# Attention, MLP and gated MLP on one core: the memory term by halves of the rows, one scores tile fewer, and another order at both ends of the second MLP

## What is computed

```python
def _attn_ref(q, k, v, M_prev, z_prev, beta):        # B, H, S, D = 4, 8, 576, 64
    scores = (1 / sqrt(D)) * q @ k.T, masked above the diagonal
    a = exp(scores - scores.max(-1)); a /= a.sum(-1) + 1e-9
    local = a @ v
    q_p = np.where(q > 0, q, np.exp(q) - 1.0) + 1.0    # phi(q)
    mem_out = (q_p @ M_prev) / (q_p @ z_prev + 1e-6)
    g = 1 / (1 + exp(-beta))                           # one gate per head
    return g * mem_out + (1 - g) * local
def _moe_ref(x, w_in, w_out):                          # 2304 tokens, 512 -> 2048 -> 512
    h = x @ w_in
    return (h / (1 + exp(-h))) @ w_out
def _moe2_ref(x, w_in, w_out, g_ln):                   # 512 -> 1024 -> 512
    h = x @ w_in
    solu = h * softmax(h)
    ln = (solu - mean) / sqrt(var + 1e-6) * g_ln
    return ln @ w_out
```

## Time and profile before

| | |
|---|---|
| runs, us | 891.49, 893.80, 893.99 |
| the profiled execution, us | 890.32 |
| its span, first to last instruction, us | 888.5 |
| mean granted clock of TensorE | 0.975 |
| PE busy, 4736 matmuls | 844.1 us, 95% |
| DVE, ACT, POOL busy | 529.3, 407.2, 340.2 us |
| hardware DMA queue, share of 16 engines | 34.9% |
| chain that ended last | PE 64%, issue 26%, ACT 4%, DVE 3% |

### The profile page before, as it was taken

How to read it: one execution, slowest core, us unless ns; L and a number is a source line. 1 busy time by engine, 2 the same in 40 slices (tenths; PEclk the granted TensorE clock), 3 DMA queues, 4 the chain that set the end, 5 groups by cost and what they waited for, 6 DMA issues and landing times.

```text
span 888.5 us, 13414 instructions
## 1 busy us (share of the span) xinstructions
PE 844.1 (95%) x4736; PEld 719.4 (81%) x4736; DVE 529.3 (60%) x1034; ACT 407.2 (46%) x897; POOL 340.2 (38%) x350
## 2 busy tenths in 40 slices
PE   4877899999999999999999999999998999999997
PEld 2665788888788888788888889999996888888885
DVE  5888776776764656665565441244435666666663
ACT  4776667666656545555554434415201222222221
POOL 4777558657645455455364314223200000000000
PEclk8898699999999999999999999999999999999998
DMA  5222265676664445445534337333200000000000
GB/s 171 82 71 71 85 208 181 219 241 221 225 200 152 146 158 163 149 146 173 176 120 135 141 122 306 120 128 134 94 1 13 24 14 21 24 24 24 24 24 24
DMA packets 50888, 105.64 MB, mean 119 GB/s; under 512 B 10384, under 2 KB 21648, under 8 KB 50576
## 3 DMA queue, kind: packets, MB, share of 16 engines
q1 hardware_dynamic: 50384, 104.88, 34.9%
q10 hardware_dynamic: 448, 0.02, 0.0%
HBM read 83.39 MB, written 21.50 MB: 118 GB/s over the span
## 4 chain that ended last, share of the span: by engine, by line
PE 64%; issue 26%; ACT 4%; DVE 3%; POOL 1%; DMA 1%; SPq 0%; POOLq 0%; ACTq 0%
PE banks L1274 23%; PE banks L1286 21%; PE banks L1242 8%; PE banks L1223 5%; PE banks L1189 4%; ACT prob L693 2%; PE banks L1197 1%; PE banks L1192 1%; ACT pt_hi L699 1%; PE banks L1400 1%; DVE pt_lo L947 1%; POOL st L675 1%; DVE neg_max L930 1%; DMA z_row<-in_z_prev 1%; ACT x_half L705 0%
## 5 line engine op out<-in xcount | busy, mean ns | idle before, releaser
L1286 PE MATMUL banks<-g_hi,wr 128*128 128x512 f32 (+1 forms) x640 | 196.6, 375 | 2.0 <-POOL g_lo L619 1.1
L602 POOL TENSOR_SCALAR prob<-prob,inv_sum,gate_all 128x576 f32<-128x576 f32 (+2 forms) x144 | 109.7, 771 | 86.9 <-DVE inv_sum L941 86.9
L1286 PEld LDWEIGHTS banks<-g_hi,wr 128*128 128x128 f32 x640 | 118.5, 188 | 17.1 <-issue 2.9
L1274 PE MATMUL banks<-xc_hi,wr 128*128 128x512 f32 x384 | 128.9, 402 | 0.0
L947 DVE TENSOR_TENSOR pt_lo<-banks,pt_hi 128x512 fp32r<-128x512 f32 x144 | 85.1, 595 | 56.4 <-ACT pt_hi L699 55.8
L1286 PE MATMUL banks<-g_lo,wr 128*128 128x512 f32 (+1 forms) x320 | 117.7, 368 | 0.0
L619 POOL TENSOR_TENSOR g_lo<-gu,g_hi 128x512 fp32r<-128x512 f32 x48 | 62.1, 1293 | 90.6 <-ACT g_hi L739 90.4
L699 ACT ACTIVATE pt_hi<-banks 128x512 fp32r<-128x512 f32 x144 | 75.6, 526 | 41.2 <-PE banks L1223 39.6
L1242 PE MATMUL banks<-pt_hi,vm 128*128 128x320 f32 (+4 forms) x352 | 90.5, 289 | 4.1 <-DVE pt_lo L947 2.2
L675 POOL TENSOR_TENSOR st<-st 128x1 f32<-128x1 f32 x18 | 9.9, 551 | 217.3 <-DVE st L1120 217.3
L693 ACT ACTIVATE prob<-banks,neg_max 128x576 f32<-128x576 f32 (+2 forms) x144 | 78.2, 548 | 19.1 <-DVE neg_max L930 14.7
(11 more groups left out here) (119 smaller groups left out, 1784.2 us busy)
## 6 DMA issues: line engine op xcount, KB each, us to landing
wr<-split_w SPq DMA_DIRECT2D x96, 512.0 KB, 3.2
split_w<-wr SPq DMA_DIRECT2D x32, 512.0 KB, 4.0
k_raw<-in_k_t SPq DMA_DIRECT2D x16, 288.0 KB, 3.1
qn_raw<-in_q_n SPq DMA_DIRECT2D x16, 288.0 KB, 3.6
out<-o SPq DMA_DIRECT2D x18, 256.0 KB, 2.0
q_raw<-in_q_t SPq DMA_DIRECT2D x16, 256.0 KB, 2.7
vm_raw<-in_v_main SPq DMA_DIRECT2D x16, 256.0 KB, 2.5
wr_raw<-in_w_in SPq DMA_DIRECT2D x16, 256.0 KB, 3.1
```

The source lines that it names most:

```text
L602: pool.tensor_scalar(pr, pr, inv_sum[p % 2][:, columns(t, h)], gate, ALU.mult, ALU.mult).then_inc(prob_done, 1)
L1274: mm = pe.matmul(out_bank, w[:, a, k], x[:, k], start=(i == 0), stop=(i == 3 * KC - 1))
L1286: mm = pe.matmul(out_bank, w[:, a, k], g, start=(i == 0), stop=(i == 11))
```

## The change

Three things are changed, and small ones that follow from them.

1. **phi by the memory.** phi(q) is laid out with head 0 of a block's 64 tokens beside head 1, even blocks of tokens in rows 0 to 63 and odd ones in rows 64 to 127 (`qn_raw[P, 5, 2, D]`; five column blocks where 4.5 are filled, loaded by four DMAs in pieces of 256 bytes). Turned, the two heads lie on the two halves of the rows, as a third head of `pt_hi` and `pt_lo`; M is in one block of `vm` (11 blocks of 64 columns in place of 14). In `values` calls 0 and 2 first make the memory product of both heads, with 64 rows each, into both banks; the heads' own products add to it. Call 0 and call 2 so wait for both banks.
2. **Scores of tiles 1 and 0** are made in one go in step 5, tile 0 behind tile 1 in the same banks, with one mask product over 256 columns; `sums` takes both at once. Step 7 has no scores.
3. **Second MLP.** `EARLY` is 29 in place of 30. The wait for the first MLP's additions stands in `turn_ln(0)`, behind the first half of `hidden2(1)`. For the last tiles (n = 17) PE does hidden2(17) ahead of product(15), and turn_ln(16) between its halves.
4. In the alone stage PE turns a step's further units ahead of `values`; `TURN` has units 1 and 2 in step 6. `v_high` goes from step 7 to 8, both `v_low` to step 9, `q_high` from 3 to 1, `k_low` and `load_qk` from 6 to 5. The first two DMAs of the tail of q are issued by ACT's queue, beta by one DMA.

```diff
-SCORES = {0: 4, 1: 3, 3: 2, 5: 1, 7: 0}
-TILES = [4, 3, 2, 1, 0]
+SCORES = {0: 4, 1: 3, 3: 2, 5: 1}
+TILES = [4, 3, 2, 1]
-TURN = [[], [-3], [], [-2], [-1], [0], [1], [2, 3], [4, 5]]
+TURN = [[], [-3], [], [-2], [-1], [0], [1, 2], [3], [4, 5]]
-EARLY = 30
+EARLY = 29
...
             def load_qn(p):
                 if p:
-                    sp.wait_ge(norm_sum, p)
+                    sp.wait_ge(phi_sum, p)
+                    sp.wait_ge(phi_z, p)
+                else:
+                    sp.wait_ge(qn_zeroed, 1)
-                sp.dma_start(qn_raw[:], q_n[i]).then_inc(qn_in, 16)
                 for h in range(2):
-                    sp.dma_start(z_row[h * D:(h + 1) * D], z_prev[i:i + 1, h, :].broadcast_to([D, D])).then_inc(qn_in, 16)
+                    for par in range(2):
+                        sp.dma_start(qn_raw[par * D:(par + 1) * D, 0:5 - par, h], q_n[i, h * D:(h + 1) * D, par::2])\
+                            .then_inc(qn_in, 16)
+                sp.dma_start(z_row[:], z_prev[i:i + 1].rearrange("o h d -> o (h d)").broadcast_to([P, 2 * D])).then_inc(qn_in, 16)
...
             def scores(p, t):
-                    w = P * (t + 1)
-                    for n, (q, k) in enumerate(products):
-                        for h in range(2):
-                            r = slice(h * D, (h + 1) * D)
-                            pe.matmul(bank[b + h][:, 0:w], q[r, P * t:P * (t + 1)], k[r, 0:w], start=(n == 0), stop=False,
-                                      skip_group_check=True)
+                    for u, at in ((t, 0),) if t > 1 else ((1, 0), (0, 2 * P)):
+                        w = P * (u + 1)
+                        for n, (q, k) in enumerate(products):
+                            for h in range(2):
+                                r = slice(h * D, (h + 1) * D)
+                                pe.matmul(bank[b + h][:, at:at + w], q[r, P * u:P * (u + 1)], k[r, 0:w],
+                                          start=(n == 0 and u == t), stop=False, skip_group_check=True)
...
             def values(p, i):
                 h = i % 2
-                if i == 0:
-                    pe.wait_ge(v_split, 2 * p + 2)
                 if h == 0:
+                    pe.wait_ge(v_split, 2 * p + 2)
                     pe.wait_ge(pt_lo_done, NU * p + VALUES_NEED[i // 2])
-                if 4 * p + i >= 2:
-                    pe.wait_ge(x_done, 4 * p + i - 1)
+                    pe.wait_ge(x_done, 4 * p + i)
+                    for pt in (pt_hi, pt_lo):
+                        for g in range(2):
+                            r = slice(g * D, (g + 1) * D)
+                            pe.matmul(bank[VALUE_BANKS[g]][:, 0:n], vm[r, 10].rearrange("p s d -> p (s d)"),
+                                      pt[r, 2, PHI_AT + first:PHI_AT + end], start=(pt is pt_hi), stop=False, skip_group_check=True)
...
-                if i < 2:
-                    product(4, 2, 3, 5, PHI_AT + 2)
-                    product(5, 2, 2, 6, PHI_AT + 2).then_inc(pv_done, 1)
-                else:
-                    product(0, 2, 2, 5, PHI_AT)
-                    product(1, 2, 2, 6, PHI_AT).then_inc(pv_done, 1)
...
             def turn_ln(n, par, first=False):
                 pe.wait_ge(ln_done, n + 1)
-                if not first:
+                if first:
+                    pe.wait_ge(y_first, firsts(BALL - 1))
+                    pe.wait_ge(y_added, adds(BALL - 1))
+                    pe.wait_ge(w2o_split, NF2)
+                else:
                     pe.wait_ge(lnt_split, 2 * n)
...
-            tile2(NTILE - 2, 0)
-            tile2(NTILE - 1, 1, last=True)
+            n = NTILE - 1
+            tile2(n - 3, 0)
+            hidden2(n - 1, 0, 0)
+            turn_ln(n - 2, 1)
+            hidden2(n - 1, 0, 1)
+            hidden2(n, 1, 0)
+            hidden2(n, 1, 1)
+            product(n - 2, 1, (0,))
+            turn_ln(n - 1, 0)
+            product(n - 2, 1, (1,))
+            product(n - 1, 0)
+            turn_ln(n, 1)
+            product(n, 1)
```

313 lines of the change are left out of this document (178 added, 135 removed).

## The result

| | before | after |
|---|---|---|
| median of four runs each, us | 893.89 | 881.36 |
| lowest and highest | 891.49, 895.16 | 878.63, 883.23 |
| the profiled execution, us | 890.32 | 878.63 |
| its span, us | 888.5 | 876.8 |

A forecast was written before the change was run, and what follows sets the result against it. PE was taken to bound the woven stage and most of the second MLP, no engine the alone stage. 11.0 + 2.2 + 4.5 + 4.7 + 4.8 + 0 = 27.2 us off 893.8 gave 866.6 us, range 858 to 879.

The forecast's parts named there:

- the prediction's own signs of being wrong: PE waits in values for POOL's vm, woven period falling under 0.8 us, or an alone pair still at 18 us.
- Part 1: Woven stage, memory product in paired 64-row matmuls: 0.92 us saved a pair, 11.0 us over 12 pairs.
- the second rival: The memory product's 64-row pairs don't overlap, so its saving vanishes: 877.6 us, chance 0.04.
- Part 2: Scores of tiles 1 and 0 made together: some 0.2 us less a pair, 2.2 us in all.
- the phi transposes: Narrower transposes of phi on PE: priced at nothing, at most 0.05 us a pair.
- Part 3: Alone stage, 4.5 pairs: 1.0 us less a pair, 4.5 us in all, bounds 0 and 9.
- The PE part of it: Alone stage: 1.0 us a pair taken from between 0 and 2, since transposes now stand ahead of values.
- the first rival: Only PE's own work goes; alone stage stays as long, clock falls at both second-MLP places: 875.6 us, chance 0.19.
- Part 4: Into the second MLP: tile 0's transposes at 670.0 in place of 674.76, 4.7 us, with a new 0.3 to 0.5 wait.
- Part 5: Program's end, new order of the last tiles: end at 880.3 against 885.06, 4.8 us, at full clock.
- Part 6: Program's start, first operation on phi and q_n's four DMAs: zero change, bounds 1 us either way.
- The slower rival: Low half of vm comes too late, PE stands 2.6 us in each of 12 pairs: 897.8 us, chance 0.05.

The follow-up runs named there:

- a2: Changed kernel with M's two heads in two vm blocks, zeros in other rows, memory products of 128 rows: four woven pairs 138.00 us, median 882.28 (0.9875).
- b6: Changed kernel with tile 1's masks ahead of tile 0's scores, so two 64-row score blocks again: four woven pairs 140.00 us, median 881.65 (0.9856).
- a1: Changed kernel with phi's last part transposed with all 128 rows, not 64: four woven pairs 138.00 us, median 878.05 (0.9843).
- f1: Changed kernel, new PE order, plus unused PE matmuls in the first head's bank: 87.7 us from pair 1 to pair 5, median 875.77 us.
- f2: f1 with PE's old alone-stage order, values ahead of second and third transposes: 86.8 us from pair 1 to pair 5, median 875.06 us.
- a3: Changed kernel with the load of q_n one step earlier on SP, ahead of load_v: 89.6 us from pair 1 to pair 5, median 878.11 (0.984).
- a4: Changed kernel with q_n's unused rows zeroed by a DVE memset at the start, not an ACT copy: median 879.15 us (0.9852).
- d2: d_all_start plus unused PE matmuls from pair 1 on, in the first head's bank: 83.5 us from pair 1 to pair 5, 865.72 us (0.9696).
- e1: Kernel before with only PE's new alone-stage order, second and third transposes ahead of values: 97.7 us from pair 1 to pair 5, median 894.66 (1.001).
- c1: Changed kernel with tile 3's first unit (30) transposed in step 7 again, not 6: 92.6 us from pair 1 to pair 5, median 883.64 us.
- d_all_start: Changed kernel with the edits of a1, a2, a3, a4, and gate, first two row maxima and first exponential ahead of phi: 870.07 us (0.9744).

## Why the prediction was wrong, step by step

Two of the prediction's own signs of being wrong came: the woven period fell by 0.60 us, less than 0.8, and a pair alone still takes 18.3.

- **Part 1, memory product (11.0).** The block was priced right to 0.01 us (0.93 for 0.92), and the pairs overlap, so the second rival is out. The step that failed is the one that priced the block alone, with nothing for its neighbours. The earlier trace rows show what the first and the last 64-row pair pay; I took that for the whole switch. The 128-row matmul behind pays as well (0.26 and 0.22 us for 0.14 and 0.12), and the masks ahead (0.21 and 0.32 us). Against the same products with all rows that is 0.49 us a pair (a2). Against the kernel before it is 0.39, and nearly all of it stands ahead, for there the first product behind the mask was costly already. So M won 0.53 us a pair by the timeline, where 0.92 was forecast. Subtraction gives about the same: of the 0.60 us that a woven pair won, 0.33 is the merged scores (b6) and -0.18 the transpose (a1), which leaves 0.45. The Trainium skill's rule ("TensorEngine Tiling (Array Packing)", Key Properties) that a change of mode drains the engine is what all this looks like (0.49 us a pair on the neighbours in a2's comparison); I had counted it within the blocks and not at their outer edges.
- **Part 2, scores (2.2) and the phi transposes (0).** The merge gave 0.33 a pair, not 0.2: the outer edges were left out here too, this time to the kernel's good, for the MLP matmul ahead of tile 0's block had paid 0.09. "A 64-row one brings its own switch" was written and then priced at nothing; it costs 0.18 a pair. Together 0.15 for 0.2.
- **Part 3, alone (4.5).** It came to nothing. "The PE part of it" was a guess between 0 and 9, and the order of PE, its main ground, shows no gain at nearly equal clock (f1, f2). What the runs show in its place is a stage of rings of nearly the same length: a3 cuts one, and the stretch goes from 90.0 to 89.6 us. In addition the clock stood at half level for 34 us and not for 23; how much of the missing 5.3 us that is stays open. This was the first rival's ground ("the clock of 0.65 at the alone stage's end, which less PE work does not raise"); I gave it 0.19, and it was right on this term and wrong on both ends of the second MLP.
- **Part 4 (4.7).** Right: the new wait is 0.40 us, forecast 0.3 to 0.5, and nothing stands ahead of the transposes.
- **Part 5 (4.8).** Right: 4.9 us, at full clock.
- **Part 6, start (0, bounds 1).** +3.3 us. I wrote "q_n comes in four DMAs behind a wait for ACT" and did not follow it. ACT's copy stood behind the table load, which needs no data and had been free; then 2.7 us of issues, then z. The trace of the kernel before had the table load (1.28 us) and one issue of q_n (0.59 us). Moving the pad off ACT gave 1.2 us back (a4).
- **The slower rival.** vm's late low half did wait in the alone stage, 0.8 us in all, and never in the woven one.

The sum, by stretch: 3.3 at the start, 5.3 alone, 7.0 in the woven pairs and what follows them up to the transposes, and -0.1 at the end make up the 15.5 us between 27.2 and 11.7.

Open: what of d2's edits takes the alone stage from about 87 to 83.5 us at nearly full clock (a3 is the nearest guess, and was not run with fill alone); why e1 at 0.76 lost 8.5 us and c1 at 0.76 only 2.6; and 0.1 us of the transposes' time a pair.

## What to carry to other kernels

Price a switch of TensorE between half and all rows at its outer edges too, here 0.1 to 0.2 us ahead of a block and 0.1 behind it; eight plain matmuls with zeros beat eight packed ones here by 0.19 us a pair. In a stage in which no engine is full, take no gain from removed work unless a row shows the wait that goes. Compare versions there only at equal clock, and know first how far one version repeats. And follow an early wait at a program's start through its queue: here 2.9 us of wait and 2.7 us of issues made the first row maximum 2.9 us late, and 3.3 us were lost by pair 1.

## What the hardware showed that I had not expected

- Adding unused matmuls to PE made kernels faster. It is clear of noise for the kernel before: 5.5 us in the median, ten runs against nineteen (0.9937, 0.9918 to 0.9957). For the changed kernel (ratios 0.9789 to 0.9808 with them, 0.986 without) and for d_all_start (0.9696 for 0.9744) it is likely: the intervals overlap. The idle time of an engine that waits for others is not free if its clock falls: busy PE time in the stretch went down from 73.42 to 72.47 us with 45 matmuls more.
- Runs of one kernel differ by more than 1%, and the clock in the alone stage is the likely cause, though no run separates it. In one round of nineteen runs of the kernel before, those with a mean clock of 0.979 to 0.983 took 888.9 to 893.0 us, those with 0.967 to 0.973 took 893.6 to 897.0. The profiled execution of e1_before_order, with 47 us at half level, took 899.05 us, 4.4 more than the kernel's median, and its ten runs went from 889.46 to 899.66 us. Four pairs with few waits (pair 10 to pair 14) repeat to 0.1 us between kernels with the same woven work.
- A 64-row transpose of 64 columns costs more than a 128-row one of 128 columns, 0.41 for 0.25 us with the matmul ahead of it.
